# A mixture-of-experts kernel with a seven-tap mix: taps as one product and one sum per column, eight output tiles, three columns scattered per tile

## The chip, the cores and the metric

One core of a Trainium2 chip. The metric is the device time of one execution of the whole program in microseconds (us).

## The reference

There are two stages. The first mixes each row of `x` (4 x 3584 rows of 192) with the six rows ahead of it, with weights from a softmax over seven taps, per row and head (8 heads of 24 columns). The second routes each mixed row to its best two of eight experts and adds the two results, weighted by a softmax of the two logits:

```python
w = softmax(weight_gen, over the 7 taps)              # B, S, H, K
out = np.einsum('bshk,bskhg->bshg', w, x_unf)         # x_unf: 7 shifted copies of x

logits = x @ w_gate
noisy_logits = logits + np.log1p(np.exp(x @ w_noise)) * noise
top2 = np.argpartition(-noisy_logits, 2, axis=1)[:, :2]
h = np.maximum(x[mask] @ w1[e], 0.0)                  # 192 -> 1024
out[mask] += top2_w[mask, k, None] * (h @ w2[e])      # 1024 -> 192
```

## The kernel before, in words

A partition holds 112 consecutive rows of `x` ("columns"). The mix runs in 14 chunks of eight columns (`C`, `CHUNKS`). A mixed chunk is routed (transposes, logits, top two, ranks within the experts), and its 8 x 128 rows are scattered twice, once per chosen expert, to a list sorted by expert in DRAM (`sorted_rows`), by indirect DMAs of GpSimd, one per column and choice (`scatter`, L390). The expert stage takes 256 rows of one expert at a time from this list, 119 tiles: SyncE loads a tile (`load_rows`, L316), TensorE transposes it, multiplies with `w1` (`up`), ScalarE takes the high half of the hidden (L521) and VectorE the low half (`low_hidden`, L886), TensorE multiplies with `w2` (`down`), ScalarE writes the output tile (`output_rows`, L532) and GpSimd adds it to the output by two indirect DMAs (`add_tile`, L401).

The first three chunks are mixed before the expert stage (`products_alone`), with the sum over taps on TensorE. The other eleven are mixed and routed beside the tiles, one chunk to each group of eight tiles. A tile has four slots, one to each pair of hidden blocks, so a chunk has 32 slots (`SLOTS`). What stands beside the tiles is put in order by hand. On ScalarE and TensorE the constants `AT_...` name the slot: the high half of a mixed chunk, `high_rows` (L491), stands in slot 23, ahead of the output of that tile; the ranks are in slot 8; the rows for the next tile are transposed in the first slot of a tile, so those of the next group in slot 28. On VectorE the routing's seven parts stand in slots 0, 1, 3, 4, 5, 7 and 8, and `beside` (L967) hands out the rest: each slot adds `SLOT_US` (1.45) to what is owed, each routing part takes its own price off, and then parts follow while anything is owed, each taking off the price that it yields. These parts are, in order: the chunk's taps (`taps`, L804, from slot 0), the lay-out of the next eight tiles (`lay_out`, L687, from slot 14; its fourth part, L718 to L720, writes the table of row and expert of each tile), `low_rows` (from 24), and for the next chunk `shift_w` (from 25), `scale_x` and `normalise_w` (from 31). `normalise_w` leaves the weights of a chunk in PSUM (`psTaps`, 64 x 7).

`taps` before works on the whole chunk, 1536 elements at a time: a product for each of seven taps (`product`, L657; x in a row, the weight of one tap broadcast over 24 columns) and six sums (L822) into `y`, with two buffers `prod`.

GpSimd takes the tiles in order. Behind the two output DMAs of a tile it scatters `SEND_COLS` columns of the chunk being routed, from the group's second tile (`SEND_FROM`), and then waits until the output DMAs have landed and frees the tile (`tile_added`, L411). After the last column `sent` (L394) waits for the scatters and tells SyncE. SyncE loads a tile eight ahead (`XB`) when its buffer is free, and the first tile of a group only when the table is written and the chunk sent (L337, L338); ahead of tile 96 it also writes nine blocks of padding rows (`write_pads`). ScalarE writes into one of `NB` output tiles and waits until the tile `NB` before is added (L529).

Of the kernel before, what the change touches and what calls it, by code (L numbers as in the profile page):

```python
# [27 lines left out]
P = 128  # L28
# [6 lines left out]
C = 8  # L35
# [24 lines left out]
NB = 4  # L60
# [18 lines left out]
SEND_FROM, SEND_COLS = 1, 2  # L79
SLOT_US = 1.45  # L80

# [11 lines left out]
def build(nc, x, wgen, wgate, wnoise, noise, w1, w2, out):  # L93
    ctx = ExitStack()
    with ctx:
# [28 lines left out]
        late = sb("late", [P, C * D + NB * TH * D], F32)  # L124
        y = late[:, 0:C * D].rearrange("p (c d) -> p c d", c=C)
        xb = [late[:, 0:(C + HALO) * D] if n == 1 else xb[:, :] for n in range(CHUNKS)]
        prod = [sb(f"prod{i}", [P, C * D], F32) for i in range(2)]
# [58 lines left out]
        yo = [late[:, C * D + i * TH * D:C * D + (i + 1) * TH * D].rearrange("p (s d) -> p s d", s=TH) for i in range(NB)]  # L186
# [426 lines left out]
        def _(dve):  # L613
# [178 lines left out]
            def products_alone(n):  # L792


                for k in range(K):
                    if n * K + k >= 2:
                        dve.wait_ge(prod_used, n * K + k - 1)
                    product(n, k, prod[(n * K + k) % 2][:, :]).then_inc(prod_ready, 1)
                    if k == K - 1:
                        dve.wait_ge(prod_ready, (n + 1) * K)  # L800
                        dve.sem_inc(taps_done, 1)
                    yield

            def taps(n):  # L804


                acc = y[:, :, :].rearrange("p c d -> p (c d)")
                if n == ALONE:
                    dve.wait_ge(prod_used, ALONE * K)
                product_at = {}  # L810
                for k in (1, 2):
                    product_at[k] = ch.put(product(n, k, prod[k % 2][:, :]))
                    yield 1.67
                sum_at = ch.put(product(n, 0, acc))
                yield 1.67
                for k in range(1, K):
                    if k == K - 1:
                        dve.wait_ge(taps_done, n + 1)
                        ch.wait(sum_at)
                    else:  # L820
                        ch.wait(max(product_at[k], sum_at))
                    add = v.tensor_tensor(acc, acc, prod[k % 2][:, :], ALU.add)  # L822
                    if k == K - 1:
                        add.then_inc(mixed, 1)
                    else:
                        sum_at = ch.put(add)
                    yield 1.67
                    if k + 2 < K:

                        ch.wait(sum_at)  # L830
                        ins = product(n, k + 2, prod[k % 2][:, :])
                        if k + 2 == K - 1:
                            ins.then_inc(taps_done, 1)
                        else:
                            product_at[k + 2] = ch.put(ins)
                        yield 1.67
# [363 lines left out]
```

## Time and profile before

| | us |
|---|---|
| runs, median of 3 | 1355.69 |
| lowest, highest | 1352.51, 1356.91 |
| profiled execution, device time | 1340.02 |
| its span in the profile | 1338.1 |

| engine | busy, us | share of the span |
|---|---|---|
| TensorE (PE), matmuls | 1159.4 | 87% |
| VectorE (DVE) | 884.8 | 66% |
| GpSimd (POOL) | 723.4 | 54% |
| ScalarE (ACT) | 657.0 | 49% |

The profile is of one execution. Its span runs from the first instruction to the last; 1.9 us of its device time lie around it. The expert stage begins near 205 us. The granted TensorE clock is 2.4 GHz in nearly all of it. Matmuls are pipelined, so a busy PE is not PE at its peak. Group g of eight tiles carries the taps of chunk 3 + g; groups 0 to 10 do, group 11 has only the last chunk's routing and scatters, and the tiles from 96 on have nothing beside them.

### The profile page before, as it was taken

To read this page: it belongs to the slowest core of one execution; us is meant where nothing else is said; L and a number is where in the kernel's file an instruction comes from. 1 tells how busy PE (TensorE), PEld (TensorE's weight loads), DVE (VectorE), ACT (ScalarE), POOL (GpSimd) and SP (SyncE) were. 2 spreads that over 40 slices of the span, in tenths; PEclk is the share of its full clock that TensorE was granted. 3 is DMA by queue.
4 is the path that set the end of the run, shared out by engine and by line. 5 is a ranking of instruction groups with operands and counts; after the bars stand their busy time and mean duration, and the time that the engine had idled before them with its cause. 6 is when DMAs were issued, how large, how long until landed. Compare 5 with 4: busy or idle time off the path is not lost.

```text
span 1338.1 us, 35681 instructions
## 1 busy us (share of the span) xinstructions
PE 1159.4 (87%) x12139; PEld 1040.7 (78%) x12139; DVE 884.8 (66%) x1732; ACT 657.0 (49%) x1120; POOL 723.4 (54%) x506
## 2 busy tenths in 40 slices
PE   4464419899999999999999999989999987999996
PEld 2222118889898999888898989989998976999996
DVE  5776817869697886869687786959787532333332
ACT  5446314454545546464555547464645532444442
POOL 3347532747566474746556574846656462333333
PEclk9786759999999999999999999999999998999998
DMA  7654652442535344442534344443533325333322
GB/s 255 194 169 150 200 164 44 98 88 50 117 66 129 54 98 85 101 92 50 129 54 119 64 101 82 98 85 57 127 52 84 56 57 118 50 47 50 48 25 25
DMA packets 110751, 124.79 MB, mean 93 GB/s; under 512 B 11372, under 2 KB 102788, under 8 KB 108928
## 3 DMA queue, kind: packets, MB, share of 16 engines
q0 software_dynamic: 45024, 46.59, 22.0%
q1 hardware_dynamic: 65568, 75.92, 19.8%
q8 instruction: 119, 1.95, 0.6%
q14 instruction: 40, 0.33, 0.1%
HBM read 62.82 MB, written 60.22 MB: 92 GB/s over the span
## 4 chain that ended last, share of the span: by engine, by line
PE 64%; POOL 11%; DVE 9%; issue 6%; DMA 6%; ACT 3%; SPq 1%; another core or an unknown queue 0%; DVEq 0%; ACTq 0%; POOLq 0%
PE psum L1106 9%; PE psum L1108 9%; PE psum L1109 9%; PE psum L1093 6%; PE psum L1089 6%; POOL sorted_rows L390 6%; PE psum L1090 6%; PE psum L1091 6%; PE psum L1092 6%; POOL out_rows L401 4%; DMA st<-sorted_rows 2%; PE psum L1078 2%; DVE prod L657 2%; DVE w2s L684 2%; PE psum L1034 1%
## 5 line engine op out<-in xcount | busy, mean ns | idle before, releaser
L401 POOL DMA_INDIRECT out_rows<-late,st x238 | 389.9, 1638 | 461.4 <-ACT late L532 329.9
L886 DVE SCALAR_TENSOR_TENSOR hidden<-psum,hidden 128x512 f16<-128x512 f32 x476 | 327.1, 688 | 364.4 <-ACT hidden L521 340.0
L521 ACT ACTIVATE hidden<-psum 128x512 f16<-128x512 f32 x476 | 282.0, 596 | 458.2 <-PE psum L1093 411.2
L1106 PE MATMUL psum<-w2s,hidden 128*128 x1904 | 469.1, 246 | 26.8 <-ACT late L532 26.1
L1109 PE MATMUL psum<-w2s,hidden 128*128 x1904 | 468.9, 246 | 0.9 <-issue 0.9
L1108 PE MATMUL psum<-w2s,hidden 128*128 x1904 | 469.1, 246 | 0.4 <-issue 0.4
L1089 PE MATMUL psum<-xT,w1s 128*128 128x256 f16 x952 | 260.4, 274 | 3.9 <-ACT xT L517 3.2
L1090 PE MATMUL psum<-xT,w1s 128*128 128x256 f16 x952 | 260.3, 273 | 0.0
L1091 PE MATMUL psum<-xT,w1s 128*128 128x256 f16 x952 | 260.2, 273 | 0.0
L1092 PE MATMUL psum<-xT,w1s 128*128 128x256 f16 x952 | 260.1, 273 | 0.0
L1093 PE MATMUL psum<-xT,w1s 128*128 128x256 f16 x952 | 260.1, 273 | 0.0
L1106 PEld LDWEIGHTS psum<-w2s,hidden 128*128 128x128 f16 x1904 | 186.3, 98 | 36.2 <-issue 32.1
L1108 PEld LDWEIGHTS psum<-w2s,hidden 128*128 128x128 f16 x1904 | 186.3, 98 | 5.0
L1109 PEld LDWEIGHTS psum<-w2s,hidden 128*128 128x128 f16 x1904 | 186.4, 98 | 0.6 <-issue 0.6
L390 POOL DMA_INDIRECT sorted_rows<-rows,pos x112 | 134.5, 1201 | 36.5 <-issue 32.4
L657 DVE TENSOR_TENSOR prod<-xb,psum 128x1536 f32<-128x1536 f32 x80 | 139.3, 1744 | 1.4 <-issue 1.2
L390 POOL DMA_INDIRECT sorted_rows<-st,pos x96 | 119.2, 1242 | 30.2 <-issue 26.2
L517 ACT ACTIVATE xT<-psum 128x768 f16<-128x768 f16 x119 | 96.6, 811 | 43.6 <-PE psum L1078 38.1
L1013 PE MATMUL psum<-prod,identf 128*128 128x512 f32 x126 | 73.1, 733 | 49.1 <-DVE prod L657 46.3
L822 DVE TENSOR_TENSOR late<-late,prod 128x1536 f32<-128x1536 f32 x66 | 115.6, 1751 | 0.0
L1089 PEld LDWEIGHTS psum<-xT,w1s 128*128 x952 | 93.3, 98 | 12.7 <-issue 5.8
L1091 PEld LDWEIGHTS psum<-xT,w1s 128*128 x952 | 93.4, 98 | 11.8
(171 smaller groups left out, 1280.9 us busy)
## 6 DMA issues: line engine op xcount, KB each, us to landing
st<-sorted_rows SPq DMA_DIRECT2D x119, 202.0 KB, 3.5
xb<-in_x SPq DMA_DIRECT2D x12, 1344.0 KB
out_rows<-zeros SPq DMA_DIRECT2D x19, 576.0 KB
st<-in_moe_w SPq DMA_DIRECT2D x8, 768.0 KB, 8.2
out_rows<-late,st POOLq DMA_INDIRECT x238
wb<-in_weight_gen SPq DMA_DIRECT2D x14, 224.0 KB
st<-in_moe_w SPq DMA_DIRECT2D x4, 512.0 KB
st<-in_moe_w SPq DMA_DIRECT2D x8, 256.0 KB
```

The source lines that it names most:

```text
L390: pool.indirect_dma_start(out=xs[0:E * RPE, :], out_offset=bass.IndirectOffsetOnAxis(ap=pos[n % 2][k][:, c:c + 1], axis=0), in_=rows[n][:, ...
L401: pool.indirect_dma_start(out=out, out_offset=bass.IndirectOffsetOnAxis(ap=xr[t % XB][:, s, D + E:D + E + 1].bitcast(I32), axis=0), in_=yo ...
L521: act.activation(hh[:, 2 * q:2 * q + 2, :].rearrange("p j t -> p (j t)"), psH[q][:, :], ACT.Relu).then_inc(hh_ready, 1)
L886: v.scalar_tensor_tensor(hl[:, hq, :].rearrange("p j t -> p (j t)"), psH[q][:, :], 0.0, hh[:, hq, :].rearrange("p j t -> p (j t)"), ALU.ma ...
L1089: nc.tensor.matmul(o, col(0), xa, start=True, stop=False)
L1090: nc.tensor.matmul(o, col(0), xc, start=False, stop=False)
L1091: nc.tensor.matmul(o, col(1), xa, start=False, stop=False)
L1092: nc.tensor.matmul(o, col(2), xbx, start=False, stop=False)
L1093: last = nc.tensor.matmul(o, col(3), xbx, start=False, stop=True)
L1106: nc.tensor.matmul(o, hh[:, j, hs], hi, start=(j == 0 and s == 0), stop=False, skip_group_check=True)
L1108: nc.tensor.matmul(o, hh[:, j, hs], lo, start=False, stop=False, skip_group_check=True)
L1109: last = nc.tensor.matmul(o, hl[:, j, hs], hi, start=False, stop=end, skip_group_check=True)
```

## The change

For each of the eight columns of a chunk, VectorE makes one product of all seven taps, 8 heads x 24 x 7 = 1344 elements, taps innermost (x read with a step of 192 floats, the weights from PSUM broadcast over the 24 columns), and one sum over the seven taps into `y`. All use one buffer, `tapped`, and each of these instructions is followed by a wait for its own end (`link`). The planner is told 1.4 us for each of the 16 instead of 1.67 for each of 13. The rest of the memory of `prod` holds four more output tiles, eight in all. The scatters go three columns to a tile: three, three and two, in three tiles of a group instead of four.

```diff
-NB = 4
+NB, LATE_NB = 8, 4
-SEND_FROM, SEND_COLS = 1, 2
+SEND_FROM, SEND_COLS = 1, 3
 SLOT_US = 1.45
+TAP_US = 1.4
...
-        late = sb("late", [P, C * D + NB * TH * D], F32)
+        late = sb("late", [P, C * D + LATE_NB * TH * D], F32)
...
-        prod = [sb(f"prod{i}", [P, C * D], F32) for i in range(2)]
+        prods = sb("prods", [P, 2 * C * D], F32)
+        prod = [prods[:, i * C * D:(i + 1) * C * D] for i in range(2)]
+        tapped = prods[:, 0:D * K]
...
-        yo = [late[:, C * D + i * TH * D:C * D + (i + 1) * TH * D].rearrange("p (s d) -> p s d", s=TH) for i in range(NB)]
+        yo = [flat[:, i * TH * D:(i + 1) * TH * D].rearrange("p (s d) -> p s d", s=TH) for flat, n in (
+            (late[:, C * D:], LATE_NB), (prods[:, D * K:], NB - LATE_NB)) for i in range(n)]
...
             def taps(n):
-                acc = y[:, :, :].rearrange("p c d -> p (c d)")
                 if n == ALONE:
                     dve.wait_ge(prod_used, ALONE * K)
-                product_at = {}
-                for k in (1, 2):
-                    product_at[k] = ch.put(product(n, k, prod[k % 2][:, :]))
-                    yield 1.67
-                sum_at = ch.put(product(n, 0, acc))
-                yield 1.67
-                for k in range(1, K):
-                    if k == K - 1:
+                for c in range(C):
+                    made = v.tensor_tensor(tapped.rearrange("p (h g k) -> p h g k", h=H, k=K),
+                                           xb[n][:, c * D:(c + K) * D].rearrange("p (k h g) -> p h g k", k=K, h=H),
+                                           psTaps[:, c * H:(c + 1) * H, :].unsqueeze(2).broadcast_to([P, H, G, K]),
+                                           ALU.mult)
+                    if c == C - 1:
+                        made.then_inc(taps_done, 1)
                         dve.wait_ge(taps_done, n + 1)
-                        ch.wait(sum_at)
                     else:
-                        ch.wait(max(product_at[k], sum_at))
-                    add = v.tensor_tensor(acc, acc, prod[k % 2][:, :], ALU.add)
-                    if k == K - 1:
-                        add.then_inc(mixed, 1)
+                        ch.link(made)
+                    yield TAP_US
+                    summed = v.tensor_reduce(y[:, c, :], tapped.rearrange("p (d k) -> p d k", k=K), AX.X, ALU.add)
+                    if c == C - 1:
+                        summed.then_inc(mixed, 1)
                     else:
-                        sum_at = ch.put(add)
-                    yield 1.67
-                    if k + 2 < K:
-
-                        ch.wait(sum_at)
-                        ins = product(n, k + 2, prod[k % 2][:, :])
-                        if k + 2 == K - 1:
-                            ins.then_inc(taps_done, 1)
-                        else:
-                            product_at[k + 2] = ch.put(ins)
-                        yield 1.67
+                        ch.link(summed)
+                    yield TAP_US
```

## Rows read from the trace of the kernel before

**Rows 1.** The page, first part: busy us, share of the span, instructions.

```profile
PE 1159.4 (87%) x12139; PEld 1040.7 (78%) x12139; DVE 884.8 (66%) x1732; ACT 657.0 (49%) x1120; POOL 723.4 (54%) x506
```

**Rows 2.** By windows: length; PE, PEld, DVE, ACT, POOL busy; clock; DMA share; GB/s.

```profile
673.00:749.00 76.00, 72.38 (x809) 67.00 (x807) 59.39 (x122) 40.84 (x73) 48.29 (x32) 1.00 0.41 86
...
1139.00:1208.00 69.00, 69.00 (x751) 65.40 (x750) 23.11 (x41) 30.47 (x56) 24.85 (x16) 1.00 0.32 47
```

**Rows 3.** Waits from 205 to 1332, PE and ACT: us in total, times, longest.

```profile
PE psum L1106 <- ACT late L532: 26.1, 24, 3.2
PE psum L1078 <- DMA st<-sorted_rows: 14.0, 6, 8.2
...
ACT late L532 <- PE psum L1109: 30.4, 73, 2.4
```

**Rows 4.** Timeline: slot 23 of one chunk, one tile of the tail: start, length.

```profile
416.44 1.48 ACT L491 ACTIVATE st<-late 128x1536 f16<-128x1536 f32 x1 [0.83 <-DVE late L822]
...
1216.86 0.73 ACT L532 ACTIVATE late<-psum,gsel 128x192 f32<-128x192 f32 x2 [0.39 <-PE psum L1109]
...
1221.00 0.69 DVE L886 SCALAR_TENSOR_TENSOR hidden<-psum,hidden 128x512 f16<-128x512 f32 x1 [1.73 <-ACT hidden L521]
...
1224.34 0.25 PE L1106 MATMUL psum<-w2s,hidden 128*128 x1
...
1225.53 0.73 ACT L532 ACTIVATE late<-psum,gsel 128x192 f32<-128x192 f32 x2 [0.39 <-PE psum L1109]
```

**Rows 5.** By windows, DVE alone, slots 10 to 21 of the third group: length, busy.

```profile
384.20:411.53 27.33, 25.69 (x30) 1.00 0.37 78
```

**Rows 6.** DVE by line and shape: count; busy us, mean ns; idle before.

```profile
L886 DVE SCALAR_TENSOR_TENSOR hidden<-psum,hidden 128x512 f16<-128x512 f32 x476 | 327.1, 688 | 364.4 <-ACT hidden L521 340.0 <-issue 21.5
L657 DVE TENSOR_TENSOR prod<-xb,psum 128x1536 f32<-128x1536 f32 x80 | 139.3, 1744 | 1.4 <-issue 1.2
L822 DVE TENSOR_TENSOR late<-late,prod 128x1536 f32<-128x1536 f32 x66 | 115.6, 1751 | 0.0
L684 DVE SCALAR_TENSOR_TENSOR w2s<-st,wscale,w2s 128x1536 f16<-128x1536 f32 x8 | 24.6, 3071 | 3.7 <-ACT w2s L469 3.6
...
L645 DVE TENSOR_REDUCE wred<-wb 128x64 f32<-128x448 f32 x14 | 8.7, 620 | 0.5
...
L733 DVE TENSOR_REDUCE lg<-psum 128x128 f32<-128x384 f32 x14 | 7.7, 546 | 0.0
...
L783 DVE TENSOR_REDUCE mr<-t 128x8 f32<-128x64 f32 x28 | 6.2, 220 | 1.0
...
L786 DVE TENSOR_REDUCE msum<-mask 128x8 f32<-128x64 f16 x14 | 3.7, 265 | 0.5
```

**Rows 7.** Timeline of POOL: a scatter beside L822, and the last routed group.

```profile
388.55 2.31 POOL L390 DMA_INDIRECT sorted_rows<-rows,pos  x1 [0.30 <-issue]
...
1061.00 1.55 POOL L401 DMA_INDIRECT out_rows<-late,st  x1 [5.25 <-ACT late L532]
...
1064.88 0.99 POOL L390 DMA_INDIRECT sorted_rows<-st,pos  x1 [0.47 <-DVE pos L784]
...
1071.79 1.61 POOL L401 DMA_INDIRECT out_rows<-late,st  x1 [2.10 <-ACT late L532]
...
1103.91 1.61 POOL L401 DMA_INDIRECT out_rows<-late,st  x1 [2.20 <-ACT late L532]
```

**Rows 8.** The chain that ended last, pieces in order of time: start, length.

```profile
725.12 3.30 DMA sorted_rows<-rows,pos
...
729.24 2.56 DMA st<-sorted_rows
...
1112.95 4.05 DMA sorted_rows<-pads
```

**Rows 9.** Timeline: the table of a group, and the transposes of tile 96.

```profile
720.73 0.17 DVE L718 TENSOR_SCALAR rowt<-base 128x8 int32<-128x8 f32 x1
...
1120.26 0.82 PE L1078 MATMUL psum<-identh,st 128*128 128x128 f16 x6 [8.24 <-DMA st<-sorted_rows]
```

More of the change, by code:

```diff
@@ L797, in products_alone @@
                         dve.wait_ge(prod_used, n * K + k - 1)
-                    product(n, k, prod[(n * K + k) % 2][:, :]).then_inc(prod_ready, 1)
+                    product(n, k, prod[(n * K + k) % 2]).then_inc(prod_ready, 1)
                     if k == K - 1:
```

## The prediction

> **What bounds the kernel now.** The page's first part comes first: TensorE (PE) is busy for 87% of the span [rows 1], far above every other engine. The view by windows then says where that is not the end of it. A stretch of eight tiles in the middle, which carries one chunk's taps, routing and scatters, takes about 76 us; eight tiles near the end, which carry none of this, take 69.3 (8 x 8.66, the step from one output activation to the next [rows 4]; the window shown is 69.0 [rows 2]). So a chunk costs some 6.5 us beside its eight tiles, and PE is the bound at 8.66 us a tile. VectorE (DVE) is busy 59.4 of 76 us there against 23.1 in the tail [rows 2]: it is the fullest engine after PE. The waits of PE in the main stage are small: 26.1 us in 24 pieces for the output activation (L532), and 14.0 us in 6 pieces for gathered rows (L1078), of which one alone is 8.2 [rows 3]. These two lines are nearly all that can be won.
>
> **How tight DVE is.** In the tail the low half of the hidden (L886) starts at 1221.00, takes 0.69, and its products start on PE at 1224.34 [rows 4]: DVE may come 2.65 us late before PE waits. In a chunk, slots 10 to 21 (three tiles, 26.0 us unstalled) took 27.33 us, with DVE busy 25.69 of them [rows 5]. And in slot 23 ScalarE (ACT) waited 0.83 us for the last sum of the taps (L491 behind L822) [rows 4]. There is little room for more DVE time in exactly the slots that the change edits.
>
> **The taps, part by part.** Removed per chunk, for 11 chunks: seven products and six sums of 1536 elements, 1744 and 1751 ns each [rows 6], 13 pieces, 22.7 us. Added: eight products of 8x24x7 = 1344 elements and eight sums that reduce 1344 to 192. A whole operation costs about 0.145 us and 1.042 ns an element: L645, a sum over seven like the new one, took 620 ns for 448 elements [rows 6], so the new sum takes 1400 + 150 = 1545 ns. The product is the disputed price. Its x operand is read with seven taps innermost, 192 floats apart. Lower bound: an element a cycle as L657, 1400 + 145 = 1545 ns. The only DVE read of SBUF in this trace with a stride from element to element is L786 (64 halves, 16 bytes apart): 265 ns against 220 for L783, the same count read in a row [rows 6], so 45 ns for 64 elements, 0.70 ns each. For 1344 that is 0.94 us, and the product 2.49 us. Upper bound: two cycles an element, the rate at which L684 ran on average, 3071 ns for 1536 (with GpSimd beside it in the setup, a distant row) [rows 6]: 2.94 us. I take 2.49, since its row has the like access. Nor below 1545: no fp32 product of DVE ran faster than an element a cycle.
>
> The Trainium skill ("Advanced Engine Details and Errata", SBUF Cachelines) says that two accesses must fall in one 16-byte line for full speed, and that a different line at every access is penalised. It gives no figure. By it the new product is slow, by "no penalty" it is not. Row L786 agrees with it; L733, which reads PSUM 64 bytes apart, shows no penalty (546 ns for 384 elements) [rows 6].
>
> Each new piece is followed at once by a wait on its own end (one buffer for the products), where the old pieces let the next instruction overlap by about 0.08 us. I put 0.04 us on each. So a product costs 2.53 and a sum 1.585; before, a piece cost 1.67.
>
> **Where they land.** The planner adds 1.45 owed per slot and subtracts 1.4 per piece. Followed from the second chunk on: pieces 0 and 1 in slots 1 and 2, 2 in slot 6, 3 to 15 in slots 10 to 21; before, 0 and 1 in slots 1 and 2, then 2 to 12 in slots 9 to 21. The last sum stays in slot 21, but the lay-out moves back: the table (L718) goes from slot 23 to 25.
> Slots 10 to 21 then hold 7 sums (11.1), 6 products (15.2), and 12 L886 at 0.61 (688 ns less the overlap) with three gates (7.6): 33.9 us. The third product, between the route parts, brings 0.9 more. Less the 2.65 that DVE may be late: 32.2 us, against 27.33 now, so +4.9. Slots 22 to 28 follow with DVE still at its limit: four lay-out parts, the low rows, L491 waiting longer, and the table two slots nearer the transposes of slot 28; an estimate of +1.6, from the 0.83 wait of L491 and one lay-out part of about 0.8. In all +6.5 us a chunk, x 11 = +71.
>
> **The scatters.** Nothing is removed: 16 indirect DMAs a chunk, each 0.99 plus 0.30 us on GpSimd (POOL) [rows 7], but in three tiles. In the last routed group the tiles' output DMAs began at 1061.00, 1071.79 and, after the fourth batch of scatters, at 1103.91 [rows 7]. With three columns: first scatter 1064.88, six of them to 1072.6, then twice 3.8 us of output DMAs, six and four more scatters: 1093.8, plus 2.3 for landing (the chain has 3.30 from a scatter's start [rows 8]), 1096, not 1103.9. Here PE lost its 8.2 us: rows sent, nine pads written (last landed 1117.0 [rows 8]), tile 96 transposed from 1120.26 [rows 9]. The pads come 8 us earlier: -8.2. In the middle groups the same path (scatter lands 728.4, load 729.24 to 731.80 [rows 8]) costs the other 14.0 - 8.2 = 5.8 us. That goes too if the table is early; with DVE late it is late next (L718 at 720.73 [rows 9] plus two slots, 4.2, plus DVE's lag 2.65, is 727.6, then 3.3 for the load). I count 0 of it. The old sums over two SBUF buffers also stretched scatters: L390 took 2.31 instead of 0.99 beside an L822 [rows 7]. That stops, and lets POOL keep up; it is on no path of its own.
>
> **Eight output tiles.** ACT's outputs waited 30.4 us in all for PE [rows 3], and next to nothing is left that a freed tile could have released. Six scatters make POOL's tile 3.8 + 7.7 = 11.5 us, against 10.7, so it falls a tile behind at most; four buffers would hold. Worth 0. The setup keeps its pieces: 0.
>
> **Sum.** +71 - 8 = +63 on the profiled execution's 1340.0: 1403. That execution lies 15.7 us below the median of the runs, so I add the same step to 1355.7: 1419.
>
> **Rivals.** First, the strided read is free (as in L733). Then slots 10 to 21 hold 20.6 + 7.6 = 28.2 us, within 26.0 + 2.65; DVE costs at most 0.5 a chunk for the late lay-out, +5.5. The scatters give -8.2 - 5.8. Together -8.5: 1347, faster by 0.6%. It decides where the product lies under about 1.9 us: below that DVE's extra is hidden. For it: L733; against it: L786.
> Second, the full two cycles: 0.45 x 8 = 3.6 us more a chunk, +40: 1459.
> Third, the burst of scatters. In the last routed group, without taps, a tile with four scatters takes 10.7 us and not 8.66 [rows 7], a stall of ACT with no releaser in the profile. If it follows the length of a burst, two tiles get 2.6 longer and one loses 2.0: +3.1 x 12 = +37, with the free read 1384. If it follows the number of tiles, it gives back 2.0 x 12 = 24. I take neither.
>
> **How the numbers follow.** Row's price 0.36, two cycles 0.24, free read 0.32, burst 0.08. What a measurement can tell from no change is 0.3%, 4 us: 1351.6 to 1359.8. Of the free read 0.27 is faster and 0.05 within; of the others 0.02 is within, the rest slower. Range: 1340 (free read, part of the burst stall gone) to 1460 (two cycles); the slow read alone would be 1385 to 1460.
>
> **What would show it.** The product's row: 2.5 us right, 1.55 the first rival, 2.9 the second. With 2.5: DVE near 69 us a chunk, chunks near 82, and PE's waits for L886 in slots 13 to 21 of each chunk; L491 waiting in most chunks. The wait of L1078 of 8.2 us gone or under 1. L390 at 0.97 on average and last scatters 8 us earlier in the last routed group. I am wrong if the chunks stay at 76 us, or if PE's new waits are for ACT's outputs or for gathered rows.

## The result, and the profile after

The changed kernel takes 1520.54 us (median of 4 runs, 1518.03 to 1522.45), the kernel before 1354.1 on the same chip (4 runs, 1345.51 to 1356.91): ratio 1.124, interval 1.1185 to 1.1295. The forecast had the direction, slower, but 1419 with a range to 1460; the time lies 60 us above that range. The profiled execution spans 1516.2 us against 1338.1.

The page of the changed kernel, first part, answers to [rows 1], and the granted clock in 40 slices follows it.

```profile
PE 1247.0 (82%) x12139; PEld 1062.9 (70%) x12139; DVE 998.7 (66%) x1765; ACT 658.4 (43%) x1120; POOL 656.5 (43%) x506
...
PEclk9676679998989999898998989989899899999999
```

The sum of TensorE's busy time is 88 us larger (1247.0 against 1159.4) for the same 12139 matmuls, and its share is down to 82%: the clock is not fully granted in most chunks (the eights and nines that alternate in the second row).

Groups of DVE and of POOL by line and shape (L814 is the new product, L824 the new sum, L879 the low half of the hidden, L394 the scatters), against [rows 6] and the scatters of before:

```profile
L879 DVE SCALAR_TENSOR_TENSOR hidden<-psum,hidden 128x512 f16<-128x512 f32 x476 | 328.6, 690 | 424.9 <-ACT hidden L525 307.0 <-issue 110.7 <-DVE macch L792 0.3
L814 DVE TENSOR_TENSOR prods<-xb,psum 128x1344 f32<-128x1344 f32 x88 | 218.9, 2488 | 0.4
L824 DVE TENSOR_REDUCE late<-prods 128x192 f32<-128x1344 f32 x88 | 135.8, 1543 | 0.0
```

```profile
L394 POOL DMA_INDIRECT sorted_rows<-rows,pos x112 | 109.3, 976 | 47.7 <-issue 32.0 <-DVE pos L788 15.5 <-DVE late L843 0.2
L394 POOL DMA_INDIRECT sorted_rows<-st,pos x96 | 93.3, 972 | 42.1 <-issue 27.4 <-DVE pos L788 14.6
```

```profile
L390 POOL DMA_INDIRECT sorted_rows<-rows,pos x112 | 134.5, 1201 | 36.5 <-issue 32.4 <-DVE pos L784 3.3 <-DMA out_rows<-late,st 0.6
L390 POOL DMA_INDIRECT sorted_rows<-st,pos x96 | 119.2, 1242 | 30.2 <-issue 26.2 <-DVE pos L784 2.8 <-DMA out_rows<-late,st 1.2
```

The product takes 2.488 us (forecast 2.49), the sum 1.543 (forecast 1.545), and a scatter is down from 1.201 and 1.242 us to 0.976 and 0.972 (forecast 0.97). These prices are not what failed.

The waits of the main stage (205 to 1510), beside [rows 3], are where the surprise is. Total, times, longest, in us:

```profile
ACT hidden L525 <- PE psum L1086: 416.6, 325, 4.3
...
ACT hidden L525 <- remote: 171.2, 41, 7.2
DVE hidden L879 <- issue: 110.7, 26, 8.0
...
PE psum L1099 <- ACT prods L536: 28.3, 23, 4.3
PE psum L1101 <- issue: 25.3, 36, 1.2
...
PE psum L1099 <- DVE hidden L879: 15.8, 27, 1.9
```

The forecast expected PE to wait for DVE (L879). It does, for 15.8 us; it waits longer, 28.3 and 7.1 us, for ACT's outputs (L536, against 26.1 before). But ACT has 171.2 us of idle time that ended on "remote", which is the profile's word where it finds no releaser on this core, and DVE and PE have pieces of "issue", idle time without any wait. The steps from one output activation (L536) to the next say where. Third group of eight tiles (one chunk):

| us | 1 | 2 | 3 | 4 | 5 | 6 | 7 | 8 | sum |
|---|---|---|---|---|---|---|---|---|---|
| before | 8.66 | 9.11 | 10.05 | 8.38 | 8.66 | 10.60 | 10.22 | 9.60 | 75.3 |
| after | 8.66 | 9.99 | 9.71 | 21.43 | 10.83 | 11.19 | 10.38 | 9.61 | 91.8 |

One step, the fourth, is 13.05 us longer, and the fourth is as long (21.1 to 22.0) in each of the ten middle groups. ACT's timeline in it, and the windows of all engines over parts of it and over the whole step (length; PE, PEld, DVE, ACT, POOL busy; granted clock; DMA share; GB/s):

```profile
422.71 0.73 ACT L536 ACTIVATE late<-psum,gsel 128x192 f32<-128x192 f32 x2 [1.29 <-PE psum L1102]
428.49 0.60 ACT L525 ACTIVATE hidden<-psum 128x512 f16<-128x512 f32 x1 [5.05 <-remote]
429.95 0.81 ACT L521 ACTIVATE xT<-psum 128x768 f16<-128x768 f16 x1 [0.86 <-remote]
437.22 0.60 ACT L525 ACTIVATE hidden<-psum 128x512 f16<-128x512 f32 x1 [6.46 <-remote]
...
444.14 0.73 ACT L536 ACTIVATE late<-psum,gsel 128x192 f32<-128x192 f32 x2 [1.32 <-PE psum L1102]
```

```profile
424.00:428.00 4.00, 2.56 (x23) 1.64 (x20) 2.43 (x2) 0.00 (x0) 3.08 (x4) 1.00 0.28 94
428.00:432.00 4.00, 1.62 (x12) 1.01 (x12) 2.15 (x2) 1.41 (x2) 3.39 (x3) 0.90 0.38 38
432.00:436.00 4.00, 3.04 (x15) 1.64 (x14) 0.00 (x0) 0.00 (x0) 3.09 (x4) 0.50 0.37 95
436.00:440.00 4.00, 1.99 (x10) 0.97 (x9) 1.97 (x3) 0.60 (x1) 2.04 (x3) 0.50 0.23 80
440.00:445.00 5.00, 4.90 (x27) 3.96 (x27) 4.93 (x5) 1.93 (x4) 0.17 (x1) 0.51 0.00 0
...
422.71:444.14 21.43, 14.54 (x94) 9.77 (x93) 11.88 (x12) 3.93 (x8) 12.59 (x12) 0.70 0.25 63
```

From 424 to 440 PE, ACT and DVE all do little; DVE and ACT have not one instruction from 432 to 436, while PE goes on in short bursts, with gaps of up to 1 us. The DMA engines are not full either (0.23 to 0.38). The one engine that keeps its rhythm is POOL, and what it issues is six scatters from 419.86 on, two output DMAs, and six scatters more, each 0.30 us behind the end of the one before:

```profile
426.24 0.96 POOL L394 DMA_INDIRECT sorted_rows<-rows,pos  x1 [0.30 <-issue]
427.51 1.61 POOL L405 DMA_INDIRECT out_rows<-late,st  x1 [0.30 <-issue]
...
431.30 1.00 POOL L394 DMA_INDIRECT sorted_rows<-rows,pos  x1 [0.30 <-issue]
...
437.68 0.97 POOL L394 DMA_INDIRECT sorted_rows<-rows,pos  x1 [0.30 <-issue]
```

```profile
429.19 0.69 DVE L879 SCALAR_TENSOR_TENSOR hidden<-psum,hidden 128x512 f16<-128x512 f32 x1 [2.77 <-issue]
...
437.92 0.69 DVE L879 SCALAR_TENSOR_TENSOR hidden<-psum,hidden 128x512 f16<-128x512 f32 x1 [6.58 <-issue]
```

At 437.92, 0.24 us after the last scatter starts, DVE resumes after 6.58 us. And in the windows from 432 to 445 the clock is granted at 0.50 or 0.51, which is 1.2 GHz, so the second half of the stall and the stretch after it are slow for PE too. This is the **stall without a releaser** that [rows 7] had shown in small (10.7 us for a tile with four scatters) and that the prediction kept out of its sum.

What it costs a group is read from DVE, which is otherwise full there. In the fourth step DVE is idle for 9.55 us (21.43 - 11.88), of which 2.77 and 6.58 are the two pieces that end at 429.19 and 437.92; in the fifth and sixth together for 0.7. Where the stall is absent (set 3 below) DVE is idle for 0.8 us in the same three steps, and the group is 9.8 us shorter.

### The profile page after: what moved, and what is told of

Same layout as the page of the kernel before. It is cut to its first block, busy times and chain, and to the rows that moved or that the text cites. A ratio compares the mean times of both kernels' runs of the same rounds, so it can differ in the third digit from the quotient of the medians.

```text
span 1516.2 us, 35868 instructions
## 1 busy us (share of the span) xinstructions
PE 1247.0 (82%) x12139; PEld 1062.9 (70%) x12139; DVE 998.7 (66%) x1765; ACT 658.4 (43%) x1120; POOL 656.5 (43%) x506
## 4 chain that ended last, share of the span: by engine, by line
DVE 40%; PE 40%; issue 11%; ACT 3%; another core or an unknown queue 2%; POOL 1%; DMA 1%; DVEq 1%; SPq 0%; ACTq 0%; POOLq 0%
DVE prods L814 11%; DVE hidden L879 7%; DVE late L824 6%; PE psum L1099 6%; PE psum L1102 6%; PE psum L1101 6%; PE psum L1086 4%; PE psum L1082 4%; PE psum L1085 4%; PE psum L1083 4%; PE psum L1084 4%; DVE prods L661 2%; PE psum L1027 1%; PE psum L1071 1%
## 5 line engine op out<-in xcount | busy, mean ns | idle before, releaser
L879 DVE SCALAR_TENSOR_TENSOR hidden<-psum,hidden 128x512 f16<-128x512 f32 x476 | 328.6, 690 | 424.9 <-ACT hidden L525 307.0
L1099 PE MATMUL psum<-w2s,hidden 128*128 x1904 | 480.6, 252 | 68.8 <-ACT prods L536 28.3
L1101 PE MATMUL psum<-w2s,hidden 128*128 x1904 | 480.5, 252 | 26.5 <-issue 25.3
L1102 PE MATMUL psum<-w2s,hidden 128*128 x1904 | 480.3, 252 | 15.6 <-issue 15.5
L405 POOL DMA_INDIRECT out_rows<-prods,st x118 | 184.8, 1566 | 354.9 <-ACT prods L536 336.9
L405 POOL DMA_INDIRECT out_rows<-late,st x120 | 188.9, 1574 | 323.0 <-ACT late L536 301.1
L1082 PE MATMUL psum<-xT,w1s 128*128 128x256 f16 x952 | 268.0, 282 | 8.6 <-issue 6.1
L1085 PE MATMUL psum<-xT,w1s 128*128 128x256 f16 x952 | 267.6, 281 | 3.4 <-issue 3.2
L1083 PE MATMUL psum<-xT,w1s 128*128 128x256 f16 x952 | 267.9, 281 | 2.5 <-issue 2.1
L1084 PE MATMUL psum<-xT,w1s 128*128 128x256 f16 x952 | 267.9, 281 | 2.0 <-issue 2.0
L1086 PE MATMUL psum<-xT,w1s 128*128 128x256 f16 x952 | 267.1, 281 | 1.7 <-issue 1.7
L814 DVE TENSOR_TENSOR prods<-xb,psum 128x1344 f32<-128x1344 f32 x88 | 218.9, 2488 | 0.4
L824 DVE TENSOR_REDUCE late<-prods 128x192 f32<-128x1344 f32 x88 | 135.8, 1543 | 0.0
L394 POOL DMA_INDIRECT sorted_rows<-rows,pos x112 | 109.3, 976 | 47.7 <-issue 32.0
L1006 PE MATMUL psum<-prods,identf 128*128 128x512 f32 x126 | 74.7, 746 | 51.5 <-DVE prods L661 46.2
L1082 PEld LDWEIGHTS psum<-xT,w1s 128*128 x952 | 95.6, 100 | 28.4 <-issue 20.3
L394 POOL DMA_INDIRECT sorted_rows<-st,pos x96 | 93.3, 972 | 42.1 <-issue 27.4
```

What stands on the lines that cost most here:

```text
L405: pool.indirect_dma_start(out=out, out_offset=bass.IndirectOffsetOnAxis(ap=xr[t % XB][:, s, D + E:D + E + 1].bitcast(I32), axis=0), in_=yo ...
L814: made = v.tensor_tensor(tapped.rearrange("p (h g k) -> p h g k", h=H, k=K), xb[n][:, c * D:(c + K) * D].rearrange("p (k h g) -> p h g k", ...
L879: v.scalar_tensor_tensor(hl[:, hq, :].rearrange("p j t -> p (j t)"), psH[q][:, :], 0.0, hh[:, hq, :].rearrange("p j t -> p (j t)"), ALU.ma ...
L1082: nc.tensor.matmul(o, col(0), xa, start=True, stop=False)
L1083: nc.tensor.matmul(o, col(0), xc, start=False, stop=False)
L1084: nc.tensor.matmul(o, col(1), xa, start=False, stop=False)
```

## Experiments

In the texts quoted, "after" is the changed kernel and a kernel named `b_...` is the kernel before with one edit. Ratios are to the kernel before on the same chip. Sets 1 to 5 ran on five different chips (that of the first pair is not on record), and that matters: in the first pair and in set 2 (kernel before 1354.1 and 1340.16) the stall is there, in sets 1, 3, 4 and 5 (1325.04, 1327.77, 1324.24, 1324.76) no kernel shows it. I call the first **stalling** and the others **calm** chips; each chip was used for one set, so that the chip and the moment cannot be told apart.

### Set 1 (calm): columns to a tile, buffers, the product's access

Back to two columns:

```diff
-SEND_FROM, SEND_COLS = 1, 3
+SEND_FROM, SEND_COLS = 1, 2
```

> The changed kernel with two columns to a tile again (four tiles with four scatters), all else kept. Two theories for the 166 us. Burst: GpSimd's six scatters in two tiles running, with the output DMAs between them, stall ScalarE, VectorE and TensorE (the fourth tile of each group takes 21.5 us where it took 8.4). It expects that tile back at 8.4 to 10 us and the run at 1390 to 1425 (before, plus the 6.5 us a chunk that was forecast for the slow product). VectorE: the stall comes from VectorE's product of 2.49 us and the wait behind each piece, and the columns only moved the place where it shows: it expects 1480 to 1530.

Measured: 1408.63 us, 1.0627 (1.0591 to 1.0664).

The kernel before, with three columns:

```diff
-SEND_FROM, SEND_COLS = 1, 2
+SEND_FROM, SEND_COLS = 1, 3
```

> The kernel before with three columns to a tile, all else kept (old taps, four output tiles). Burst: slower than before by at least 3 us a chunk (in the last routed group, which has no taps, a tile with six scatters took 13.7 us and one with four 10.7), so 1380 or more, and up to 1480 if the 13 us of the fourth tile come from scatters alone. VectorE: faster than before by the 8 us of the padding's earlier start, 1340 to 1350.

Measured: 1298.1 us, 0.9831 (0.9761 to 0.9901).

Four output tiles:

```diff
-NB, LATE_NB = 8, 4
+NB, LATE_NB = 4, 4
```

> The changed kernel with four output tiles in turn, as before (the memory stays laid out). If eight tiles are worth nothing, as forecast, the same as the changed kernel within 0.3%, 1516 to 1525. If GpSimd falls more than three tiles behind in the long stall, slower by 10 us or more. If the outputs in the new place cost something, faster.

Measured: 1406.43 us, 1.0614 (1.0579 to 1.0649).

Two columns, and the product walks its elements with x in a row and writes `tapped` seven floats apart:

```diff
-made = v.tensor_tensor(tapped.rearrange("p (h g k) -> p h g k", h=H, k=K),
-                       xb[n][...].rearrange("p (k h g) -> p h g k", k=K, h=H),
+made = v.tensor_tensor(tapped.rearrange("p (h g k) -> p k h g", h=H, k=K),
+                       xb[n][...].rearrange("p (k h g) -> p k h g", k=K, h=H),
```

> As a_cols2, and the product walks x in a row (taps outermost), with its result written 7 floats apart and the weights read from PSUM 7 floats apart. If the price of 2.49 us is that of a strided read of SBUF, the product takes 1.55 us, VectorE loses 0.94 x 8 = 7.5 us a chunk, and the run is at 1345 to 1360. If a strided write costs the same, the product stays at 2.5 us and the run equals a_cols2.

Measured: 1419.69 us, 1.0719 (1.0683 to 1.0755). The product's row:

```profile
L814 DVE TENSOR_TENSOR prods<-xb,psum 128x1344 f32<-128x1344 f32 x88 | 228.4, 2596 | 0.4
```

What follows: (a) none of these has the 166 us of the first pair, and neither has the changed kernel itself on a calm chip (set 3); (b) writing 28 bytes apart costs slightly more than reading 768 bytes apart, 2596 against 2488 ns, the second of the two outcomes expected; (c) three columns alone, on the kernel before, gain 27 us here, where the forecast had 8, and where the two theories expected 1380 or more and 1340 to 1350, against a kernel before of 1354; (d) the buffers do nothing, as far as 1406.4 here and the 1404.4 of set 3 can be compared across two calm chips.

### Set 2 (stalling): the changed kernel again, and a free product

The changed kernel, unchanged:

> The changed kernel unchanged, so that it is measured on the same chip as its variants. Burst (three columns to a tile stall the engines): 11 us or more a chunk slower than a_cols2_again, near 1520 or 1.12 of before. Chip: the stall of 13 us in the fourth tile of each group, which no variant on the other chip showed in any form, belongs to the chip that runs it, not to the code; then on a chip where the kernel before takes 1325, this one takes 1400 to 1415, the same as its variant with four output tiles (1406), and its fourth tile 8.7 us.

Measured: 1510.45 us, 1.1261 (1.1229 to 1.1294).

Two columns again, same edit as before:

> Two columns to a tile once more, beside the changed kernel. Burst: at least 100 us faster than after_again. Chip: within 10 us of it on a chip without the stall; on a chip with it, in between before and after_again. The first tiles of a group decide: 8.7 us for the fourth without the stall.

Measured: 1446.59 us, 1.0790 (1.0757 to 1.0823).

The product in rows throughout, so that the stride falls to PSUM (weights 7 floats apart) and to the sum, which reads 192 floats apart:

```diff
-made = v.tensor_tensor(tapped.rearrange("p (h g k) -> p h g k", h=H, k=K),
-                       xb[n][...].rearrange("p (k h g) -> p h g k", k=K, h=H),
-                       psTaps[...].unsqueeze(2).broadcast_to([P, H, G, K]),
+made = v.tensor_tensor(tapped.rearrange("p (k h g) -> p k h g", h=H, k=K),
+                       xb[n][...].rearrange("p (k h g) -> p k h g", k=K, h=H),
+                       psTaps[...].rearrange("p h k -> p k h").unsqueeze(3)...
...
-summed = v.tensor_reduce(y[:, c, :], tapped.rearrange("p (d k) -> p d k", k=K), AX.X, ALU.add)
+summed = v.tensor_reduce(y[:, c, :], tapped.rearrange("p (k d) -> p d k", k=K), AX.X, ALU.add)
```

> The changed kernel, with the stride moved off the product: taps outermost, so x is read and the product written in a row, the weights read from PSUM 7 floats apart; the sum then reads its 7 values 192 floats apart. Strided SBUF read costs (0.70 ns an element): product 1.55 us, sum 2.49, the time equals after_again within 0.5%. If the PSUM step is what costs: product 2.5 us and sum 2.5, some 8 us a chunk slower. If a sum reads a stride for nothing: product 1.55, sum 1.55, as a_free.

Measured: 1515.28 us, 1.1303 (1.1268 to 1.1338). The price moved from one row to the other:

```profile
L824 DVE TENSOR_REDUCE late<-prods 128x192 f32<-128x1344 f32 x88 | 216.3, 2458 | 0.0
L814 DVE TENSOR_TENSOR prods<-xb,psum 128x1344 f32<-128x1344 f32 x88 | 136.1, 1546 | 0.4
```

And a product without any stride: it reads the same 1344 floats of x in a row, so it pairs weights with other elements of x, and the convolution's result is another one.

```diff
-xb[n][...].rearrange("p (k h g) -> p h g k", k=K, h=H),
+xb[n][...].rearrange("p (h g k) -> p h g k", k=K, h=H),
```

> The changed kernel with the price of the strided read taken away: the product reads the same 1344 floats of x in a row, so each output mixes other elements of x than the reference; all else is kept. Forecast for the free read: product 1.55 us, VectorE 3.1 us a column, the chunk no slower than before, the end 8 us or more earlier: 0.985 to 1.000 of before. If the waits behind each piece, or where the pieces land, cost more than forecast, it is over 1.01.

Measured: 1459.02 us, 1.0885 (1.0851 to 1.0920), with the product at

```profile
L814 DVE TENSOR_TENSOR prods<-xb,psum 128x1344 f32<-128x1344 f32 x88 | 136.1, 1546 | 0.4
```

What follows: the wide step in SBUF costs 0.94 us in the product and 0.91 in the sum, wherever it is put, and the step of 28 bytes in PSUM nothing (1546 ns, as in the product without any stride). Taking it away gives back 51 us (1510.45 - 1459.02), but the kernel is still 119 us above the kernel before. In its trace the fourth step is still 19.67 us. The expected 0.985 to 1.000 was missed. So the stall doesn't come from the slow product. With two columns the fourth step is 12.89 us instead of 20.45 and the kernel is 64 us faster (1510.45 - 1446.59; at least 100 was expected), on a chip where the stall exists; on calm chips the same edit is worth nothing (1408.63, and 1404.37 below). DVE is idle for 3.5 us in that step and the group takes 85.3 us, 3.2 more than on a calm chip:

```profile
410.20:423.10 12.90, 11.10 (x96) 9.12 (x95) 9.43 (x9) 3.70 (x7) 8.84 (x8) 0.87 0.33 73
```

The same kernel with two columns on both kinds of chip, its last routed group, which has scatters and no taps, shows the stall by itself. Windows over five tiles and a little (41 and 47 us long, ending at like places), and the waits on "remote" in the whole main stage:

```profile
1129.00:1170.00 41.00, 41.00 (x455) 38.86 (x454) 23.43 (x74) 19.86 (x36) 28.47 (x23) 1.00 0.33 57
```

```profile
1157.00:1204.00 47.00, 42.59 (x462) 39.46 (x460) 23.77 (x74) 19.37 (x37) 28.46 (x23) 1.00 0.31 53
```

```profile
ACT hidden L525 <- remote: 48.4, 18, 4.6
...
ACT xT L521 <- remote: 3.9, 10, 0.9
```

On the calm chip PE is busy 41.00 of 41.00 us and the waits have no row with "remote". On the other it is busy 42.59 of 47.00 with the clock at full, and POOL does the same 23 instructions in 28.5 us in both. The steps between output activations in that group:

| us | 1 | 2 | 3 | 4 | 5 | 6 | 7 | 8 |
|---|---|---|---|---|---|---|---|---|
| two columns, calm | 8.66 | 8.66 | 8.90 | 8.69 | 8.66 | 8.66 | 8.66 | 19.89 |
| two columns, stalling | 8.66 | 8.66 | 10.78 | 10.65 | 10.57 | 10.58 | 8.35 | 18.59 |
| three columns (after), stalling | 8.66 | 8.66 | 13.72 | 13.73 | 10.72 | 8.49 | 8.66 | 8.66 |

Over 8.66, four scatters to a tile cost 2.1 us, six cost 5.1 us. The prediction's rival had 2.6 on top of 10.7; it is 3.0. A group has 16 scatters in either form, but the first seven steps add up to 72.6 us with three columns (71.7 in set 2) and to 68.3 with two: the length of a batch counts, and not only the number. PE is the bound in this group, so the clock is part of the price. The two steps with six scatters of the changed kernel in set 2 are nearly equal in length, the first at a clock of 1.00, the second at 0.75:

```profile
1234.54:1247.75 13.21, 10.47 (x119) 9.57 (x117) 6.75 (x22) 3.82 (x7) 8.93 (x8) 1.00 0.30 64
1247.75:1261.38 13.63, 11.76 (x89) 9.87 (x90) 4.96 (x18) 3.60 (x7) 9.01 (x8) 0.75 0.28 61
```

Against the calm steps at the same places (8.90 and 8.69) the first shows the stall alone, 4.3 us for six scatters, where four cost 1.9 and 2.0 (10.78 and 10.65, clock 1.00).

### Sets 3 to 5 (calm): the terms apart, each three times

They were meant for a stalling chip; all three sets fell on calm ones, so what was expected there of the stall stays untested. They repeat, and the repeats show how far the ratios hold.

> The changed kernel as the anchor of this set. With the stall 1.124 to 1.130 of before; on a chip without it 1.055 to 1.07, as its variants with four output tiles and with two columns had there (1.061, 1.063).

Measured: 1404.37 us, 1.0600 (1.0574 to 1.0627).

> The kernel before with three columns to a tile, once more: the first such run was on a chip without the stall (0.983 of before). On a chip with the stall (to be seen in the last routed group: tiles with four scatters at 10.7 us in a_cols2_again and in the kernel before, at 8.7 in a_cols2), two accounts differ. If the stall hangs on how many scatters follow each other, the fourth tile of a group is long here too, 15 us or more, and the run at 1.03 to 1.09 of before. If the old sums L822, which hold GpSimd's scatters up (2.3 us instead of 0.97 for those that meet one), keep the burst short, the groups gain at most 3 us each and the run is at 0.98 to 1.02. On a chip without the stall: 0.983 again.

Measured: 1308.67 us, 0.9854 (0.9794 to 0.9915).

The free product with two columns (both edits above; the same part of the computation is another one):

> Product with x in a row (other elements of x than the reference are mixed) and two columns to a tile. The two costs taken apart: on a chip with the stall a_free was 51 us under after_again, a_cols2_again 64 under it. If they add, 1.13 less 0.038 less 0.048: 1.04 of before (1395 where before takes 1340). If the forecast for the free read holds with the burst gone, 0.99 to 1.01. On a chip without the stall: 0.99 to 1.00.

Measured: 1326.47 us, 0.9998 (0.9975 to 1.0022).

The changed kernel, where the two scatters of a column wait until all those of the columns before have landed:

```diff
+                    pool.wait_ge(scattered, (routed * C + c) * 2 * 16)
                     scatter(routed, c)
```

> The changed kernel, where GpSimd waits before each column until the scatters ahead have landed, so that at most two are under way. Burst by its depth: the stall goes, the fourth tile of a group takes under 12 us instead of 20.4, and what is left are waits of TensorE for gathered rows at the end of a group, since the rows are sent some 15 us later; 1.06 to 1.10 of before on a chip with the stall. If the stall hangs on the number of scatters and not on how closely they follow: the fourth to sixth tile stay long together, 1.12 or more. On a chip without the stall: slower than after_third by the late rows, 1.06 to 1.09.

Measured: 1413.42 us, 1.0663 (1.0638 to 1.0688).

Sets 4 and 5 repeated three of them:

> The kernel before with three columns to a tile; as said for b_cols3_again, should this chip have the stall (before at 1340 or more): 1.03 to 1.09 of before if the number of scatters in a row is what counts, 0.98 to 1.02 if the old sums keep the burst short. Without the stall 0.98 to 0.99.

Measured: 1296.41 us, 0.9801 (0.9773 to 0.9830).

> The changed kernel with at most one column's scatters under way. With the stall: by closeness the fourth tile of a group falls under 12 us and the run is at 1.06 to 1.08 of before (it was 1.066 without the stall); by number it is 1.10 or more. Without the stall 1.066 again.

Measured: 1413.63 us, 1.0679 (1.0661 to 1.0697).

> Product with x in a row (other elements of x are mixed) and two columns to a tile. With the stall: 1.04 of before if the costs of product and burst add, 1.00 if the stall with four scatters in a tile is no larger than in the kernel before. Without the stall 1.000 again.

Measured: 1325.69 us, 1.0011 (0.9995 to 1.0027).

> The kernel before with three columns to a tile, for a chip with the stall: 1.03 to 1.09 of before if the number of scatters in a row counts, 0.98 to 1.02 if the old sums keep the burst short. Without the stall 0.98.

Measured: 1306.69 us, 0.9869 (0.9824 to 0.9913).

> The changed kernel with one column's scatters under way. With the stall: 1.06 to 1.08 by closeness, 1.10 or more by number. Without the stall 1.067.

Measured: 1412.78 us, 1.0646 (1.0600 to 1.0691).

> Product with x in a row (other elements of x are mixed), two columns to a tile. With the stall: 1.04 if the costs add, 1.00 if four scatters in a tile stall no more than in the kernel before. Without the stall 1.000.

Measured: 1326.53 us, 0.9999 (0.9972 to 1.0026).

The changed kernel on a calm chip: page, first part; main waits; and windows over the fourth, fifth and sixth step of the third group.

```profile
PE 1192.4 (85%) x12139; PEld 1043.6 (74%) x12139; DVE 994.6 (71%) x1765; ACT 660.5 (47%) x1120; POOL 659.7 (47%) x506
```

```profile
PE psum L1099 <- DVE hidden L879: 57.2, 67, 2.3
...
PE psum L1071 <- DMA st<-sorted_rows: 7.1, 1, 7.1
```

```profile
404.29:412.97 8.68, 8.68 (x97) 8.23 (x96) 8.51 (x8) 3.82 (x7) 7.02 (x6) 1.00 0.30 74
412.97:423.57 10.60, 9.41 (x96) 7.94 (x95) 10.39 (x10) 3.83 (x8) 8.26 (x8) 1.00 0.35 74
423.57:438.61 15.04, 11.92 (x106) 9.96 (x105) 14.66 (x17) 5.20 (x8) 7.84 (x7) 0.89 0.44 109
```

No wait on "remote" is left: PE waits for DVE (57.2 us), as the forecast said it would, and DVE is busy 33.56 of 34.3 us. In the third window the clock is granted at 0.89. PE's own timeline has the place: 1.3 us after a wait of 2.28 us ends, matmuls of one shape (L1082 to L1086) start 0.21 us apart, where they start 0.11 apart at full clock:

```profile
430.35 0.25 PE L1099 MATMUL psum<-w2s,hidden 128*128 x1 [2.28 <-DVE hidden L879]
...
431.83 0.42 PE L1083 MATMUL psum<-xT,w1s 128*128 128x256 f16 x1
432.04 0.42 PE L1084 MATMUL psum<-xT,w1s 128*128 128x256 f16 x1
```

The steps of the third group on calm chips:

| us | 1 | 2 | 3 | 4 | 5 | 6 | 7 | 8 | sum |
|---|---|---|---|---|---|---|---|---|---|
| before, three columns | 8.66 | 9.15 | 8.45 | 8.69 | 8.66 | 9.53 | 9.36 | 9.60 | 72.1 |
| after | 8.66 | 9.99 | 9.39 | 8.68 | 10.60 | 15.04 | 10.08 | 9.60 | 82.0 |
| after, two columns | 8.66 | 9.97 | 9.44 | 8.69 | 10.49 | 15.12 | 10.09 | 9.60 | 82.1 |
| free product, two columns | 8.66 | 9.03 | 8.53 | 8.69 | 8.66 | 11.28 | 10.07 | 9.60 | 74.5 |

What follows: the price of the strided read is worth 82 to 83 us with two columns (1408.63 against some 1326, and 7.6 us a chunk). With it gone the new form of the taps is not faster than the old one: with two columns in both, the ratio is 1.00. (The old form with three columns has 72.1 us a chunk against 74.5; the free product with three columns was not run on a calm chip.) With four output tiles, with eight, with two columns or three, the changed kernel is within 5 us of itself on calm chips. Spacing the scatters costs 9 us where there is no stall to save (a line lower in that kernel, so L1072 is L1071): POOL waits for them,

```profile
POOL sorted_rows L394 <- DMA sorted_rows<-st,pos: 62.2, 30, 3.8
POOL sorted_rows L394 <- DMA sorted_rows<-rows,pos: 61.8, 30, 4.0
...
PE psum L1072 <- DMA st<-sorted_rows: 15.8, 1, 15.8
```

and tile 96 gets its rows later, 15.8 us of wait instead of 7.1. What it would do on a stalling chip was not measured.

## Why the prediction was right in direction and short in size

**The product's price** was right: 2.488 against 2.49. Taking the row with the like access (L786) over the row that was merely strided (L733) decided the sign on calm chips (1.06 with it, 1.00 without it and two columns). On the stalling chip it did not: there the free product is 1.0885, so the direction would have come out with the wrong price too, which is luck. That both rows were right, each for its memory, is shown by the kernel with rows throughout: one reads SBUF, the other PSUM. The rule in the Trainium skill ("Advanced Engine Details and Errata", SBUF Cachelines), that a new 16-byte line at each access is penalised, agrees: 0.94 us on 1344 reads, and on 1344 writes 1.05. For the step in PSUM that page ("PSUM Cachelines") has lines of 8 bytes, and no penalty shows on DVE here. The rivals of the free read and of two full cycles fall by the row.

**The taps' term, +6.5 us a chunk, was mis-sized**: +9.9 (82.0 - 72.1, both with three columns, both calm). DVE's timeline shows where. In both kernels the ninth low half of the hidden opens slot 10 and the twenty-first stands behind the last piece of taps in slot 21. The kernel before with three columns, whose group has its first output activation at 364.09:

```profile
380.95 0.68 DVE L886 SCALAR_TENSOR_TENSOR hidden<-psum,hidden 128x512 f16<-128x512 f32 x1
...
405.72 0.68 DVE L886 SCALAR_TENSOR_TENSOR hidden<-psum,hidden 128x512 f16<-128x512 f32 x1
```

The changed kernel, with its first at 384.91:

```profile
403.05 0.68 DVE L879 SCALAR_TENSOR_TENSOR hidden<-psum,hidden 128x512 f16<-128x512 f32 x1
...
437.10 0.68 DVE L879 SCALAR_TENSOR_TENSOR hidden<-psum,hidden 128x512 f16<-128x512 f32 x1
```

From the one to the other it took 24.8 us and takes 34.05, for which the prediction had counted 33.9 of work: +9.3, and DVE comes to slot 10 1.3 us later (18.1 after that activation, against 16.9). So the work in slots 10 to 21 was counted well, and **the step that failed is "Less the 2.65 that DVE may be late"**. That slack was gone before slot 10: the longer product in slot 1 and the one in slot 6, where none stood before (of the early pieces the prediction counted only 0.9 us, for one), had already made the second and third step 0.8 and 0.9 us longer. And it was taken off one side only: the 27.33 that it was set against comes from a kernel whose DVE was nearly full too (25.69) and used the slack as well. Left out, the prediction's own terms give 33.9 + 0.9 - 27.33 = 7.5, with the 1.6 of the later slots 9.1 a chunk, near the 9.9. That "chunks near 82" came true on the calm chip (82.0) is luck: it was 6.5 on top of 76, and is 9.9 on top of 72.1. Of TensorE's clock: the window with 0.89 has some 3.3 us at half in 15.04 (an estimate from its mean), so 1.7 us of work a chunk, and DVE is busy 14.66 of these 15.04, so most of it lies beside DVE's work; no run separates it. Times 11 chunks the term is +109, not +71. Less what three columns give on the kernel before (18 to 28 us) that is 81 to 91, near the 76.6 measured.

**The scatters' term, -8,** missed in two ways. On the kernel before, three columns give 18 to 28 us on calm chips (four runs, 0.980 to 0.987, 95% intervals from 0.976 to 0.991), more than the 8.2 and 14.0 the prediction allowed. Where they come from isn't shown, since no trace of the unedited kernel before exists from a calm chip; tile 96's wait is not it, being still 8.2 to 9.7 us in those runs. On the changed kernel they give 0 (1.0627 and 1.0600), and tile 96's step shrinks by 2 us, from 19.89 to 17.86. The scatters of the last routed group did not end 8 us earlier: the last one starts 53.1 us into it against 57.8 in the first pair, and 48.7 against 52.5 on calm chips (the group's start being the last output activation of the group before). The prediction's 1093.8 has POOL go from tile to tile without a wait, but steps with six scatters were 13.7 us on the stalling chip. "The wait of 8.2 us gone or under 1" was wrong on calm chips (7.1). On the stalling chip it did go (last step 8.66, where two columns have 18.59); there the stalls before it give the rows 3.5 to 4.4 us more than with two columns, which may be why.

**What the sum left out** is most of the miss. On calm chips the change is worth 1.0600, 76.6 us, against the +63 forecast: a fair size, but in part by luck, since the taps were priced 38 us too low and the gain of the three columns 10 to 20 too low. On the stalling chips it is worth 166 and 170. The prediction saw the stall in [rows 7], wrote its rival as a burst with a price of 2.6 us more for a tile with six scatters (about right: 13.7 against 10.7), and then gave it 0.08 and wrote "I take neither". **The second step that failed is that**: a stall that the trace shows, with no releaser, belongs in the sum with its size for a tile, since the change edits the number of scatters in a tile. It would not have been enough: 1419 with the rival's 37 is 1456, and with the 3.5 to 4.4 us by which three columns exceed two in the last routed group, times 12, it is 1461 to 1472. Its size without taps wasn't its size with them: beside the taps the fourth step grew by 13.05 us, in ten groups by some 130, of which the sixth step gives back part (11.19 against 15.04 on a calm chip). Per chunk, 91.8 - 75.3 = 16.5 is 9.9 for the taps, 9.8 for the stall beyond them (91.8 - 82.0), less 3.2, by which the kernel before on its stalling chip stands above three columns on a calm one (75.3 - 72.1).

One of the forecast's signs of being wrong also showed in the first pair: PE's waits for ACT's outputs (28.3 + 7.1 us) are longer than those for DVE (15.8). On the calm chip it is the other way, 11.8 against 57.2.

**Why the fourth step stalls so much longer** is argued, not shown. The clock is part of how the step looks: its mean is 0.70, PE is idle for 6.9 us of it and works 9.7 us at half clock. But DVE's idle time there ends on no wait for PE and adds up to the group's loss (9.55 and 9.8), so the clock most likely explains little of the time. As for the length of the stall itself: in the kernel before the sums over two SBUF buffers (L822) held scatters up, to 1.2 us on average and up to 2.31; with them gone the scatters of the fourth tile follow each other with 0.30 us between them, twelve and two output DMAs in a row. "On no path of its own", the prediction said of that stretching; it may have been what kept the stall short. For it: in set 2 two columns, where batches are shorter, lengthen that step by 4.2 us over the calm 8.69 (12.89) and three by 11.8 (20.45). That fits the number of scatters alone as well. What would show it, the kernel before with three columns on a stalling chip, was run four times, each on a calm chip; its scatters follow each other there with 0.30 us between them (last routed group), and nothing stalls.

**Eight output tiles worth 0** stands: 1.0614 with four, 1.0600 with eight.

**Open:** what holds PE, ACT and DVE up while POOL issues; why some chips (or moments) do it and others not; whether the number of scatters or their closeness counts. Two rivals are not supported by the pages: DMA load, since the engines' share is 0.23 to 0.38 in the stall and no lower on the calm chip (0.30 to 0.44), and a larger number of packets that bring instructions, since both pages have the same 119 and 42. Whether single ones come late was not looked into.

**A better version:** the kernel before with three columns to a tile beats both on calm chips, 0.980 to 0.987 in four runs, a gain of 1.3 to 2.0%. On a stalling chip it wasn't measured, and six scatters to a tile cost 3.0 us more there in the group without taps, so it may lose.

## What to carry to other kernels

Fewer instructions aren't less time: one product and one sum in place of a chain of each need their operand in a row, or each element of SBUF read or written with a wide step costs 1.6 to 1.7 times its price; look for the row with the same memory and the same step before trusting a row that is only strided. Where the slack of a second engine hides its work, follow how late it is from the first piece on: a slack may be subtracted once, and not where earlier pieces have spent it. And a stall that no releaser explains is a term of the sum as long as the change touches what runs beside it: price it by the idle time of the engine that is full there; run the baseline on the same chip as every variant, since the same pair of kernels was 6% apart on one chip and 12.5% on another.

## What the runs showed of the hardware

- A product of two fp32 operands of 1344 elements on DVE: 1546 ns with SBUF read and written in a row, 2488 with x read 768 bytes apart, 2596 with the result written 28 bytes apart. A sum over seven of the same size: 1543 ns in a row, 2458 with its reads 768 bytes apart. A PSUM operand with a step of 28 bytes: 1546, no cost.
- Indirect DMAs issued by GpSimd about every 1.27 us come with a standstill of ScalarE and VectorE (single pieces up to 7.2 and 8.0 us in the first pair) and short gaps of TensorE (up to 1.2 us) in two of six sets, with nothing in the trace that releases them. A tile's step grows by 2.1 us for four, by 5.1 for six (4.3 where the clock stays full), and by 12 to 13 for twelve in a row beside the taps. In the four other sets, each on its chip, such kernels run at 8.66 to 8.90 us a tile.
- Such an indirect DMA takes 0.97 us on GpSimd, and 1.20 to 1.24 on average where VectorE's fp32 sums over two SBUF buffers ran beside it (2.31 for one of them).
- TensorE was granted 0.50, 1.2 GHz, 1.3 us after a wait of 2.28 us on a calm chip (0.89 in a window of 15.04 us), and from about 432 to 445 us, in and after the standstill, on the stalling one (0.70 over a step of 21.43).
